# Seven diagonal products in place of a seven-tap sum: the side channels of tiles 0 and 1, and two main taps of tile 1, move from VectorE to TensorE

## The chip, the core and the metric

The kernel is one program on one core of a Trainium2 chip. The metric is the device time of the slowest (here the only) core, in microseconds (us). The kernel before took 2252.99 us (median of 3 runs, 2252.92 to 2253.04). An engine is called by its name or by the short name of the profile: TensorE (PE, its weight loads PEld), VectorE (DVE), ScalarE (ACT), SyncE (SP, which here only issues transfers).

## The reference

`x` is (4, 4096, 192) float32. Layer 0 is a causal convolution with 7 taps, where each of 8 heads (24 channels each) has its own taps; layers 1 and 2 are two token-wise two-matrix networks with 2048 inner features.

```python
w = exp(weight - max(weight)); w = w / (sum(w) + 1e-9)      # (8 heads, 7 taps)
y0[b, s, h, g] = sum_k w[h, k] * x_padded[b, s + k, h, g]    # 6 zeros ahead of each sequence
h1 = y0 @ w_in;   y1 = (h1 * cos(h1)) @ w_out                # 192 -> 2048 -> 192
h2 = relu(y1 @ w2_in); out = (h2 * h2) @ w2_out              # 192 -> 2048 -> 192
```

## The kernel before

The 16384 tokens are 32 tiles of 512. A tile has 192 channels: 128 main channels on 128 partitions, and 64 side channels, whose 512 tokens are folded into two halves of 256 on the upper and the lower 64 partitions. So the convolution's sum of one tile is `conv`, 128 x 768: 512 columns of main channels (`conv_main`) and 256 of side channels (`conv_side`). VectorE makes it in seven instructions (`tap`): a product for tap 0, then six multiply-adds, each of which reads the one before.

TensorE works in float32r. For accuracy each operand is split into a high part and the rest (`x_hi`, `x_lo`, `up_hi`, `up_lo` and so on): ScalarE copies the high part, VectorE subtracts it to get the low part, and products high by high, high by low and low by high are summed. Inner features are taken in eight pairs of 128 per layer. Layer 1 is called "A", layer 2 "B"; a slot is one pair of one layer, and a tile has 16 slots. In a slot TensorE makes `h` (the "up" products) for this pair and adds the pair of four slots before to `y_A` or `y_B` (the "down" products). TensorE uses the upper and the lower 64 rows of its array at once, for different products, the lower ones some steps behind. `h` has two buffers, so the up products of a slot wait until ScalarE has copied `h` of the slot two before (`taken`). The down products of a pair wait for its low part (`lo_made`).

The order on each engine is written by hand, in `turns` and `body`: turn i handles layer 1 of tile i, layer 2 of tile i-1 and the convolution of tile i+1. Turn -1 is the opening: the convolution of tile 0 and the split of layer 1's first weights. Turn 0 has layer 1 alone (slots 3 to 10 hold A 0 to A 7; `FIRST_SLOTS`), with the convolution of tile 1 spread over slots 4 to 10 (`FIRST_TAP_SLOTS`). From turn 1 on both layers run; turns 3 to 30 are a hardware loop.

In an A slot VectorE does, in this order: `low_part` of the slot two before, `times_cosine` of the slot before, the tap of this slot, `fraction` (two instructions) of this slot. ScalarE does `high_part` of the slot two before, the sine (`turned_cosine`) of the slot before, and `read_h` of this slot. In turn 0, slots 11 to 15 hold only the down products of A 4 to A 7.

`on_zeros` are products with a zeroed operand into `y_B`, whose result nobody reads: 42 + 12 in the opening (`WARM_UP`; the 12 wait for the seventh tap of tile 0), and 8 each ahead of the down products of A 5 and A 6 in turn 0 (`FILL`). The sums `y_B` of layer 2 are first used in turn 1.

In the opening ScalarE splits the first part of layer 1's up weights (512 of 2048 columns), then `x` of tile 0 (`split_x1_main`, `split_x1_side`), then the second part (1536 columns). The first up product waits for VectorE's `split_x1` (`x1_made`).

Of the kernel before, what the change touches and what calls it, by code (L numbers as in the profile page):

```python
# [44 lines left out]
FIRST_TAP_SLOTS = (4, 5, 6, 7, 8, 9, 10)  # L45
# [13 lines left out]
WARM_UP, FILL = (42, 12), {5: 8, 6: 8}  # L59
# [58 lines left out]
def tile_program(nc, x, taps_in, w1i, w1o, w2i, w2o, out):  # L118
# [15 lines left out]
    with ExitStack() as ctx:  # L134
# [51 lines left out]

        stage_in_side = sb("stage_in_side", [P, F])
# [9 lines left out]
        taps_loaded = sem("taps_loaded")  # L197
        wi_loaded = (sem("wi_loaded_0"), sem("wi_loaded_1"))
# [6 lines left out]
        taps_exp = sem("taps_exp")  # L205
        wi_hi = sem("wi_hi")
        wi_lo = sem("wi_lo")
        late_hi_made = sem("late_hi_made")
        late_lo = sem("late_lo")
        even_made = sem("even_made")  # L210


# [42 lines left out]
        def _(sp):  # L255
# [33 lines left out]
            sp.wait_ge(tap_done, 2 * K)  # L289
            load_x(2)  # L290
# [19 lines left out]
        def _(pe):  # L310
# [4 lines left out]
            def up_waits(turn, s, kind, p):  # L315
# [140 lines left out]

            def body(turn):
                if turn.first:
                    pe.wait_ge(zeroed, 2)
                    on_zeros(WARM_UP[0])  # L460
                    pe.wait_ge(tap_done, K)
                    on_zeros(WARM_UP[1])
                    return
                for s, (kind, p) in enumerate(turn.slots()):
# [17 lines left out]
        def _(act):  # L482
            act.dma_start(taps[:, :], taps_in).then_inc(taps_loaded, 16)

# [4 lines left out]
            act.activation(unused[:, :], quarter[:, :], ACT.Sin)  # L489

            def layer1_hi_side(part):
                act.wait_ge(wi_loaded[part], 48)
                a, b = (0, FIRST_PART) if part == 0 else (FIRST_PART, F)
                act.activation(up_side["A"][:, a:b], stage_in_side[:, a:b], ACT.Copy).then_inc(wi_hi, 1)
                even = stage_in_side[hi_rows["A"], a:b].rearrange("p (c n m) -> p c n m", n=PAIR, m=P)
                act.activation(up_even[hi_rows["A"], a // (PAIR * P):b // (PAIR * P), :], even[:, :, 0, :], ACT.Copy)
# [80 lines left out]
            def split_x1_side(turn):  # L577

                x_side = xin_side["A"]
                act.activation(x_side[top, halves[0]], conv_side[top, :], ACT.Copy)  # L580
                act.activation(x_side[low, halves[1]], conv_side[low, :], ACT.Copy).then_inc(x1_hi, 1)
                act.activation(x_side[low, halves[0]], conv_side[top, :], ACT.Copy)
                act.activation(x_side[top, halves[1]], conv_side[low, :], ACT.Copy).then_inc(x1_hi, 1)

            def body(turn):
                if turn.first:
                    layer1_hi_side(0)
                    layer1_hi_main(0)
                    split_x1_main(turn)
                    split_x1_side(turn)  # L590
                    layer1_hi_side(1)
                    layer1_hi_main(1)
                    return
# [34 lines left out]
        def _(dve):  # L628
# [72 lines left out]
            def tap(turn, k):  # L701
                done = (turn.i + 1) * K + k
                if k == 0:
# [4 lines left out]
                    dve.tensor_scalar(conv_parts, parts[:, :, 0:HALF_TOK], taps[:, 0:1], None, ALU.mult)\  # L708
# [3 lines left out]
                dve.scalar_tensor_tensor(out=conv_parts, in0=parts[:, :, k:k + HALF_TOK], scalar=taps[:, k:k + 1],  # L712
# [114 lines left out]
```

## Time and profile before

| | |
|---|---|
| median of 3 runs | 2252.99 us |
| the profiled execution | 2253.41 us |
| its span (first to last instruction) | 2251.1 us |
| mean granted TensorE clock | 0.999 |
| TensorE busy | 2239.1 us (99%) |
| VectorE busy | 1774.6 us (79%) |
| ScalarE busy | 1734.8 us (77%) |

Busy time is the share of the span in which an engine had an instruction in work. The chain that ended last is followed back from the last instruction, from each step to what released it: it is 97% TensorE, 2% VectorE, 1% ScalarE. Of VectorE's part nearly all lies in the first 82 us. All starts below are us from the span's start.

### The profile page before, as it was taken

What the parts mean: (1) busy time and instruction counts of PE and PEld (TensorE: products, weight loads), DVE (VectorE), ACT (ScalarE), POOL (GpSimd) and SP (SyncE); (2) the same over time, 40 slices, a digit from 0 to 9 for tenths busy, and PEclk for the clock granted to TensorE, in tenths of its full rate; (3) what the DMA queues carried; (4) which work ended last, traced back from release to release, by engine and by line L of the source; (5) the groups of instructions that cost most, each with busy time, mean ns of one, the idle gap of its engine ahead of it and who ended that gap; (6) DMA issues with size and microseconds to landing.
All of it is one profiled execution on the core that took longest, in us unless ns stands there. A gap on an engine that the chain in (4) does not pass through costs nothing.

```text
span 2251.1 us, 46857 instructions
## 1 busy us (share of the span) xinstructions
PE 2239.1 (99%) x19526; PEld 2213.3 (98%) x19526; DVE 1774.6 (79%) x1813; ACT 1734.8 (77%) x1844; POOL 0.2 (0%) x4
## 2 busy tenths in 40 slices
PE   8999999999999999999999999999999999999999
PEld 7899999999999999999999999999999999999998
DVE  8887788777787777887778877778877788777773
ACT  6677777777877777777778777787777787777876
POOL 0000000000000000000000000000000000000000
PEclk9999999999999999999999999999999999999999
DMA  4000000000000000000000000000000000000000
GB/s 127 27 15 15 9 14 12 10 14 7 14 14 7 14 9 13 14 7 14 14 7 14 14 7 14 7 14 14 7 14 14 7 14 14 7 14 7 7 8 15
DMA packets 13456, 33.26 MB, mean 15 GB/s; under 512 B 1905, under 2 KB 1905, under 8 KB 13169
## 3 DMA queue, kind: packets, MB, share of 16 engines
q1 hardware_dynamic: 13280, 32.81, 4.9%
q8 instruction: 24, 0.39, 0.1%
q14 instruction: 8, 0.06, 0.0%
q10 hardware_dynamic: 144, 0.00, 0.0%
HBM read 20.22 MB, written 12.58 MB: 15 GB/s over the span
## 4 chain that ended last, share of the span: by engine, by line
PE 97%; DVE 2%; ACT 1%; issue 0%; DMA 0%
PE h L346 10%; PE h L350 10%; PE h L348 10%; PE h L352 10%; PE y_A L402 5%; PE y_A L396 5%; PE y_A L400 5%; PE y_A L398 5%; PE y_A L404 5%; PE h L355 5%; PE y_B L400 5%; PE y_B L398 5%; PE y_B L396 5%; PE y_B L404 5%; PE y_B L402 5%; DVE conv L712 0%
## 5 line engine op out<-in xcount | busy, mean ns | idle before, releaser
L698 DVE TENSOR_TENSOR g_lo<-g,g_hi 128x1024 fp32r<-128x1024 f32 x512 | 625.2, 1221 | 272.0 <-ACT g_hi L545 271.1
L545 ACT ACTIVATE g_hi<-g 128x1024 fp32r<-128x1024 f32 x512 | 538.3, 1052 | 44.1 <-DVE g L694 43.4
L537 ACT ACTIVATE w<-w,quarter 128x1024 f32<-128x1024 f32 x256 | 295.5, 1154 | 304.6 <-DVE w L688 304.6
L396 PE MATMUL y_A<-g_hi,dn_lo_A 64*128 64x512 f32 x1024 | 396.9, 388 | 0.1
L402 PE MATMUL y_A<-g_hi,dn_side_A 64*128 64x512 f32 x1024 | 396.3, 387 | 0.0
L398 PE MATMUL y_A<-g_hi,dn_hi_A 64*128 64x512 f32 x1024 | 396.0, 387 | 0.0
L400 PE MATMUL y_A<-g_lo,dn_hi_A 64*128 64x512 f32 x1024 | 395.8, 387 | 0.0
L404 PE MATMUL y_A<-g_lo,dn_side_A 64*128 64x512 f32 x1024 | 395.8, 387 | 0.0
L348 PE MATMUL h<-x_hi_A,up_lo_A 64*128 64x512 f32 x1024 | 394.5, 387 | 0.0
L352 PE MATMUL h<-x_hi_A,up_hi_A 64*128 64x512 f32 x1024 | 394.5, 386 | 0.0
L350 PE MATMUL h<-x_lo_A,up_hi_A 64*128 64x512 f32 x1024 | 394.4, 386 | 0.0
L396 PE MATMUL y_B<-g_hi,dn_lo_B 64*128 64x512 f32 x1000 | 386.6, 387 | 0.0
L398 PE MATMUL y_B<-g_hi,dn_hi_B 64*128 64x512 f32 x1000 | 386.1, 386 | 0.0
L400 PE MATMUL y_B<-g_lo,dn_hi_B 64*128 64x512 f32 x1000 | 386.0, 386 | 0.0
L404 PE MATMUL y_B<-g_lo,dn_side_B 64*128 64x512 f32 x992 | 382.9, 386 | 0.0
L402 PE MATMUL y_B<-g_hi,dn_side_B 64*128 64x512 f32 x992 | 382.9, 386 | 0.0
L352 PE MATMUL h<-x_hi_B,up_hi_B 64*128 64x512 f32 x992 | 382.9, 386 | 0.0
L348 PE MATMUL h<-x_hi_B,up_lo_B 64*128 64x512 f32 x992 | 382.9, 386 | 0.0
L350 PE MATMUL h<-x_lo_B,up_hi_B 64*128 64x512 f32 x992 | 382.9, 386 | 0.0
L694 DVE TENSOR_TENSOR g<-w,g 128x1024 f32<-128x1024 f32 x256 | 313.7, 1225 | 22.7 <-ACT w L537 1.2
L688 DVE SCALAR_TENSOR_TENSOR w<-w,g 128x1024 f32<-128x1024 f32 x256 | 313.7, 1225 | 8.8
L528 ACT ACTIVATE g<-h 128x1024 f32<-128x1024 f32 x256 | 262.2, 1024 | 70.2 <-PE h L352 59.5
(122 smaller groups left out, 6180.0 us busy)
## 6 DMA issues: line engine op xcount, KB each, us to landing
xt<-x SPq DMA_DIRECT2D x32, 393.0 KB, 3.1
out<-late SPq DMA_DIRECT2D x32, 256.0 KB, 2.0
out<-late SPq DMA_DIRECT2D x32, 128.0 KB, 2.3
late<-w_out SPq DMA_DIRECT2D x2, 1536.0 KB, 9.5
stage_in_side<-w_in SPq DMA_DIRECT2D x2, 512.0 KB, 4.2
stage_in_side<-w_in SPq DMA_DIRECT2D x4, 256.0 KB, 5.3
w<-w_in SPq DMA_DIRECT2D x1, 768.0 KB, 7.1
stage_in_side<-w_in SPq DMA_DIRECT2D x2, 384.0 KB, 9.1
```

The source lines that it names most:

```text
L348: mm = pe.matmul(dst, up_lo[kind][rows, f], x_hi[rows, :], start=False, stop=z)
L350: mm = pe.matmul(dst, up_hi[kind][rows, f], x_lo[rows, :], start=False, stop=z)
L352: mm = pe.matmul(dst, up_hi[kind][rows, f], x_hi[rows, :], start=False, stop=z)
L396: mm = pe.matmul(sums[:, 0, :], dn_lo[kind][rows, c, :], hi, start=a, stop=False)
L398: mm = pe.matmul(sums[:, 0, :], dn_hi[kind][rows, c, :], hi, start=False, stop=False)
L400: mm = pe.matmul(sums[:, 0, :], dn_hi[kind][rows, c, :], lo, start=False, stop=z)
L402: mm = pe.matmul(sums[:, 1, :], dn_side[kind][rows, c, :], hi, start=a, stop=False)
L404: mm = pe.matmul(sums[:, 1, :], dn_side[kind][rows, c, :], lo, start=False, stop=z)
L545: act.activation(g_hi[:, s % RING, :, :], g[:, s % RING, :, :], ACT.Copy).then_inc(hi_made[kind], 1)
L688: dve.scalar_tensor_tensor(out=v, in0=v, scalar=ROUND, in1=u, op0=ALU.subtract, op1=ALU.subtract).then_inc(frac, 1)
L694: dve.tensor_tensor(u, v, u, ALU.mult).then_inc(g_made, 1)
L698: dve.tensor_tensor(g_lo[:, r, :, :], g[:, r, :, :], g_hi[:, r, :, :].bitcast(F32), ALU.subtract).then_inc(lo_made[kind], 1)
```

## The change

TensorE makes part of the convolution with diagonal matrices. ScalarE, after an identity matrix has been loaded (one more transfer, 128 x 128 float32, issued by ScalarE into `y_side`), writes seven scaled copies `diag[:, k, :]`, each with tap k of every channel on its diagonal. A product of `diag[:, k, :]` with the shifted columns of `x` is tap k. These operands are plain float32, not float32r.

- Tile 0: the 256 side columns are seven such products, in TensorE's opening (`side_taps(0)`), into bank 1 of `y_B`; VectorE's seven taps cover 512 columns.
- Tile 1: the 256 side columns are seven products after the up products of slot 5 (`side_taps(1)`); taps 0 and 1 of the 512 main columns are two products after slot 6 (`main_taps`), into bank 0 of `y_B`. VectorE's taps 0 and 1 (slots 4 and 5) go; its tap 2 (slot 6, `tap_on_sums`) reads the sum in PSUM and writes `conv`; all five that are left cover 512 columns.
- Zero products in the opening: 14, then the seven side products, then 6, then (after the seventh tap) 12. `FILL` stays at 8 and 8.
- ScalarE's opening order: seven diagonal copies, then the high parts of the first weights with `up_even` last, then the side split (it waits for `conv_made`), then the main split, then the second part of the weights, again with `up_even` last. A semaphore `wi_even` covers `up_even`.

```diff
-FIRST_TAP_SLOTS = (4, 5, 6, 7, 8, 9, 10)
+PE_TAPS = 2
+FIRST_TAP_SLOTS = (None, None, 6, 7, 8, 9, 10)
-WARM_UP, FILL = (42, 12), {5: 8, 6: 8}
+WARM_UP, FILL = (14, 6, 12), {5: 8, 6: 8}
+        conv_pe, conv_pe_side = y["B"][:, 0, :], y["B"][:, 1, 0:HALF_TOK]
+        ident, diag = y_side[:, 0:P], sb("diag", [P, K, P])
             sp.wait_ge(tap_done, K)
+            sp.wait_ge(conv_made, 1)
             load_x(1)
             sp.wait_ge(wi_lo, 4)
+            sp.wait_ge(wi_even, 2)
             load_layer2_up(0)
...
+            def side_taps(t):
+                pe.wait_ge(x_loaded, (t + 1) * 16)
+                for k in range(K):
+                    if t == 0:
+                        pe.wait_ge(diag_made, k + 1)
+                    mm = pe.matmul(conv_pe_side, diag[:, k, :], parts[:, 2, k:k + HALF_TOK],
+                                   start=k == 0, stop=k == K - 1)
+                mm.then_inc(conv_made, 1)
+            def main_taps():
+                for k in range(PE_TAPS):
+                    mm = pe.matmul(conv_pe.rearrange("p (s n) -> p s n", s=2), diag[:, k, :],
+                                   parts[:, 0:2, k:k + HALF_TOK], start=k == 0, stop=k == PE_TAPS - 1)
+                mm.then_inc(conv_made, 1)
...
+                        if turn.peeled and turn.i == 0 and p == 2:
+                            side_taps(1)
+                        if turn.peeled and turn.i == 0 and p == 3:
+                            main_taps()
...
             act.dma_start(taps[:, :], taps_in).then_inc(taps_loaded, 16)
+            act.dma_start(ident, identity).then_inc(ident_loaded, 16)
...
+            act.wait_ge(ident_loaded, 16)
+            act.wait_ge(taps_step, 6)
+            for k in range(K):
+                act.activation(diag[:, k, :], ident, ACT.Copy, scale=taps[:, k:k + 1]).then_inc(diag_made, 1)
...
                 if turn.first:
                     layer1_hi_side(0)
                     layer1_hi_main(0)
+                    layer1_hi_even(0)
+                    split_x1_side(turn)
                     split_x1_main(turn)
-                    split_x1_side(turn)
...
+            def tap_on_sums():
+                k = PE_TAPS
+                dve.wait_ge(conv_made, 3)
+                dve.wait_ge(x1_hi, 3)
+                dve.wait_ge(x1_made, 1)
+                dve.scalar_tensor_tensor(out=conv_parts[:, 0:2, :], in0=parts[:, 0:2, k:k + HALF_TOK],
+                                         scalar=taps[:, k:k + 1],
+                                         in1=conv_pe.rearrange("p (s n) -> p s n", s=2),
+                                         op0=ALU.mult, op1=ALU.add).then_inc(tap_done, k + 1)
```

ScalarE, from the load of the taps to the second part of the weights. Before:

```order
L489 ACTIVATE unused<-quarter 128x1 [waits zeroed]
L494 ACTIVATE up_side_A<-stage_in_side 128x512 [waits wi_loaded_0]
L496 ACTIVATE up_even<-stage_in_side 64x256
L500 ACTIVATE up_hi_A<-w 128x512
L575 ACTIVATE x_hi_A<-conv 128x512 [waits tap_done]
L580 ACTIVATE x_side_A<-conv 64x256
L581 ACTIVATE x_side_A<-conv 64x256
L582 ACTIVATE x_side_A<-conv 64x256
L583 ACTIVATE x_side_A<-conv 64x256
L494 ACTIVATE up_side_A<-stage_in_side 128x1536 [waits wi_loaded_1]
```

The same stretch of ScalarE now (`y_side` holds the identity):

```order
L533 ACTIVATE diag<-y_side,taps 128x128 [waits taps_step,ident_loaded]
L533 ACTIVATE diag<-y_side,taps 128x128 x6
L538 ACTIVATE up_side_A<-stage_in_side 128x512 [waits wi_loaded_0]
L548 ACTIVATE up_hi_A<-w 128x512
L543 ACTIVATE up_even<-stage_in_side 64x256
L630 ACTIVATE x_side_A<-y_B 64x256 [waits conv_made]
L631 ACTIVATE x_side_A<-y_B 64x256
L632 ACTIVATE x_side_A<-y_B 64x256
L633 ACTIVATE x_side_A<-y_B 64x256
L623 ACTIVATE x_hi_A<-conv 128x512 [waits tap_done]
L538 ACTIVATE up_side_A<-stage_in_side 128x1536 [waits wi_loaded_1]
```

Seven copies stand ahead of the weights, and the side split stands ahead of the main one, behind a wait for TensorE.

TensorE in turn 0, from the last up products of slot 5 (A 2) to the first of slot 6 (A 3), before:

```order
L350 MATMUL h<-x_lo_A,up_hi_A 128x512
L352 MATMUL h<-x_hi_A,up_hi_A 128x512
L346 MATMUL h<-x_side_lo,up_side_A 128x512 [waits taken_A]
L348 MATMUL h<-x_hi_A,up_lo_A 128x512
L350 MATMUL h<-x_lo_A,up_hi_A 128x512
```

The same place of TensorE now (`diag` and `xt` are the float32 operands), and behind it the place between slot 6 and the first products of slot 7 (A 4):

```order
L367 MATMUL h<-x_lo_A,up_hi_A 128x512
L369 MATMUL h<-x_hi_A,up_hi_A 128x512
L479 MATMUL y_B<-xt,diag 128x256 [waits x_loaded]
L479 MATMUL y_B<-xt,diag 128x256 x6
L363 MATMUL h<-x_side_lo,up_side_A 128x512 [waits taken_A]
L365 MATMUL h<-x_hi_A,up_lo_A 128x512
```

```order
L369 MATMUL h<-x_hi_A,up_hi_A 128x512
L485 MATMUL y_B<-xt,diag 128x512 x2
L363 MATMUL h<-x_side_lo,up_side_A 128x512 [waits lo_made_A,late_lo,taken_A]
L413 MATMUL y_A<-g_hi,dn_lo_A 128x512
L365 MATMUL h<-x_hi_A,up_lo_A 128x512
```

Nine float32 products came in; nothing of TensorE's other work changed places.

VectorE in turn 0 at slots 4 to 6, before and now (`conv<-xt,taps` is tap 0, L712 and L767 are later taps; the instruction ahead of a tap is `times_cosine`, the one behind it starts `fraction`):

```order
L694 TENSOR_TENSOR g<-w,g 128x1024 [waits cosine]
L708 TENSOR_SCALAR conv<-xt,taps 128x768 [waits x1_made,x1_hi,x_loaded]
L686 TENSOR_SCALAR w<-g 128x1024 [waits taken_A]
L688 SCALAR_TENSOR_TENSOR w<-w,g 128x1024 [waits whole]
L663 SCALAR_TENSOR_TENSOR dn_side_A<-late,dn_side_A 128x16x64 [waits late_hi_made]
L698 TENSOR_TENSOR g_lo<-g,g_hi 128x1024 [waits hi_made_A]
L694 TENSOR_TENSOR g<-w,g 128x1024 [waits cosine]
L712 SCALAR_TENSOR_TENSOR conv<-xt,taps,conv 128x768 [waits tap_done]
L686 TENSOR_SCALAR w<-g 128x1024 [waits taken_A]
```

```order
L747 TENSOR_TENSOR g<-w,g 128x1024 [waits cosine]
L739 TENSOR_SCALAR w<-g 128x1024 [waits taken_A]
L741 SCALAR_TENSOR_TENSOR w<-w,g 128x1024 [waits whole]
L751 TENSOR_TENSOR g_lo<-g,g_hi 128x1024 [waits hi_made_A]
L747 TENSOR_TENSOR g<-w,g 128x1024 [waits cosine]
L781 SCALAR_TENSOR_TENSOR conv<-xt,taps,y_B 128x512 [waits x1_hi,x1_made,conv_made]
L739 TENSOR_SCALAR w<-g 128x1024 [waits taken_A]
L741 SCALAR_TENSOR_TENSOR w<-w,g 128x1024 [waits whole]
L751 TENSOR_TENSOR g_lo<-g,g_hi 128x1024 [waits hi_made_A]
```

The taps of slots 4 and 5 are gone, and the tap of slot 6 reads `y_B` and has 512 columns.

## Rows read from the trace of the kernel before

**Rows 1.** The page: busy time, share and count of each engine.

```profile
PE 2239.1 (99%) x19526; PEld 2213.3 (98%) x19526; DVE 1774.6 (79%) x1813; ACT 1734.8 (77%) x1844; POOL 0.2 (0%) x4
```

**Rows 2.** Windows: stretch, length, busy (count) by engine, clock, DMA share, GB/s.

```profile
0.00:5.00 5.00, 3.52 (x8) 2.81 (x9) 1.03 (x5) 1.69 (x3) 0.20 (x4) 1.00 0.55 167
...
30.00:35.00 5.00, 3.59 (x20) 3.50 (x22) 4.96 (x6) 2.15 (x3) 0.00 (x0) 0.74 0.79 285
...
100.00:110.00 10.00, 10.00 (x92) 8.27 (x90) 8.58 (x10) 8.72 (x11) 0.00 (x0) 1.00 0.00 0
```

**Rows 3.** Timeline of the opening, VectorE and ScalarE: start, duration, what [idle before <-releaser].

```profile
5.61 1.02 DVE L708 TENSOR_SCALAR conv<-xt,taps 128x768 f32<-128x768 f32 x1
6.10 0.20 ACT L489 ACTIVATE unused<-quarter 128x1 f32<-128x1 f32 x1
6.66 6.29 DVE L712 SCALAR_TENSOR_TENSOR conv<-xt,taps,conv 128x768 f32<-128x768 f32 x6
7.34 0.63 ACT L494 ACTIVATE up_side_A<-stage_in_side 128x512 fp32r<-128x512 f32 x1 [1.04 <-DMA stage_in_side<-w_in]
...
12.98 0.63 ACT L575 ACTIVATE x_hi_A<-conv 128x512 fp32r<-128x512 f32 x1 [3.92 <-DVE conv L712]
...
14.80 0.42 ACT L583 ACTIVATE x_side_A<-conv 64x256 fp32r<-64x256 f32 x1
...
15.24 1.49 ACT L494 ACTIVATE up_side_A<-stage_in_side 128x1536 fp32r<-128x1536 f32 x1
15.33 0.42 DVE L722 TENSOR_TENSOR x_side_lo<-conv,x_side_A 64x256 fp32r<-64x256 f32 x1
...
19.13 1.76 DVE L654 TENSOR_TENSOR up_lo_A<-w,up_hi_A 128x1536 fp32r<-128x1536 f32 x1 [0.61 <-ACT up_hi_A L500]
...
20.92 0.69 DVE L686 TENSOR_SCALAR w<-g 128x1024 f32<-128x1024 f32 x1
```

**Rows 4.** Tile stage_in_side: its transfers' issue times, and us to landing.

```profile
L262 SPq DMA_DIRECT2D stage_in_side<-w_in x4: 466/584/685, 1.6 to 4.0; - x4
...
DMA to landing us min/median/max: 3.8/5.2/10.0
```

**Rows 5.** Timeline of TensorE, from the last zero products to slot 7.

```profile
13.00 2.60 PEld L455 LDWEIGHTS y_B<-x_side_last 128*128 128x128 f32 x12 [0.47 <-DVE conv L712]
...
15.95 0.49 PE L346 MATMUL h<-x_side_lo,up_side_A 64*128 64x512 f32 x1
...
18.48 0.50 PE L346 MATMUL h<-x_side_lo,up_side_A 64*128 64x512 f32 x1
...
24.20 0.39 PE L352 MATMUL h<-x_hi_A,up_hi_A 64*128 64x512 f32 x1
...
31.41 0.46 PE L346 MATMUL h<-x_side_lo,up_side_A 64*128 64x512 f32 x1 [2.79 <-DVE g_lo L698]
```

**Rows 6.** Timeline of turn 0, VectorE and ScalarE, slots 7 and 8.

```profile
40.69 1.23 DVE L698 TENSOR_TENSOR g_lo<-g,g_hi 128x1024 fp32r<-128x1024 f32 x1 [0.26 <-ACT g_hi L545]
...
46.94 1.01 ACT L528 ACTIVATE g<-h 128x1024 f32<-128x1024 f32 x1
...
48.21 1.01 DVE L712 SCALAR_TENSOR_TENSOR conv<-xt,taps,conv 128x768 f32<-128x768 f32 x1
49.14 0.69 DVE L686 TENSOR_SCALAR w<-g 128x1024 f32<-128x1024 f32 x1
```

**Rows 7.** Timeline of TensorE, slot 10 to the end of turn 0's down products.

```profile
48.00 0.50 PE L346 MATMUL h<-x_side_lo,up_side_A 64*128 64x512 f32 x1 [0.74 <-ACT g L528]
...
52.66 0.49 PE L402 MATMUL y_A<-g_hi,dn_side_A 64*128 64x512 f32 x1
...
66.09 0.39 PE L400 MATMUL y_A<-g_lo,dn_hi_A 64*128 64x512 f32 x1
66.64 0.47 PE L396 MATMUL y_A<-g_hi,dn_lo_A 64*128 64x512 f32 x1
...
69.58 0.39 PE L400 MATMUL y_A<-g_lo,dn_hi_A 64*128 64x512 f32 x1
```

More of the change, by code:

```diff
@@ L115, in before, with tile_program @@
                 return None
-def tile_program(nc, x, taps_in, w1i, w1o, w2i, w2o, out):
+def tile_program(nc, x, taps_in, identity, w1i, w1o, w2i, w2o, out):
     TILES, _, WIDTH = x.shape
@@ L210, in tile_program @@
         even_made = sem("even_made")
+        conv_made = sem("conv_made")
         filled = {k: sem(f"filled_{k}") for k in "AB"}
@@ L289, in _ @@
             sp.wait_ge(tap_done, 2 * K)
+            sp.wait_ge(conv_made, 3)
             load_x(2)
@@ L577, in split_x1_side @@
             def split_x1_side(turn):
[L579 to L583, printed above, removed]
+                x_side, sums = xin_side["A"], side_sums(turn)
+                if turn.peeled and turn.i <= 0:
+                    act.wait_ge(conv_made, turn.i + 2)
+                act.activation(x_side[top, halves[0]], sums[top, :], ACT.Copy)
+                act.activation(x_side[low, halves[1]], sums[low, :], ACT.Copy).then_inc(x1_hi, 1)
+                act.activation(x_side[low, halves[0]], sums[top, :], ACT.Copy)
+                act.activation(x_side[top, halves[1]], sums[low, :], ACT.Copy).then_inc(x1_hi, 1)
             def body(turn):
@@ L707, in tap @@
                         dve.wait_ge(x1_made, turn.i + 1)
-                    dve.tensor_scalar(conv_parts, parts[:, :, 0:HALF_TOK], taps[:, 0:1], None, ALU.mult)\
+                    sums, held = conv_of(turn)
+                    dve.tensor_scalar(sums, held[:, :, 0:HALF_TOK], taps[:, 0:1], None, ALU.mult)\
                        .then_inc(tap_done, 1)
@@ L711, in tap @@
                 dve.wait_ge(tap_done, done)
[L712 to L723 removed]
+                sums, held = conv_of(turn)
@@ new lines, in tap, with conv_of @@
+                dve.scalar_tensor_tensor(out=sums, in0=held[:, :, k:k + HALF_TOK], scalar=taps[:, k:k + 1],
+                                         in1=sums, op0=ALU.mult, op1=ALU.add).then_inc(tap_done, 1)
+            def conv_of(turn):
+                n = 2 if turn.peeled and turn.i <= 0 else 3
+                return conv_parts[:, 0:n, :], parts[:, 0:n, :]
+            def tap_on_sums():
[7 more added lines that the diff above has]
+                                         op0=ALU.mult, op1=ALU.add).then_inc(tap_done, k + 1)
@@ new lines, in split_x1 @@
+            def split_x1(turn):
+                x_side, sums, to = xin_side["A"], side_sums(turn), lo_rows["A"]
+                if not turn.first:
+                    dve.wait_ge(x1_hi, turn.i * 3 + 4)
+                    dve.tensor_tensor(xin_lo["A"][:, :], conv_main, xin_hi["A"][:, :].bitcast(F32), ALU.subtract)
+                dve.wait_ge(x1_hi, turn.i * 3 + (6 if turn.peeled and turn.i == 0 else 5))
+                dve.tensor_tensor(xin_side_lo[to, halves[0]], sums[top, :],
+                                  x_side[top, halves[0]].bitcast(F32), ALU.subtract)
+                done = dve.tensor_tensor(xin_side_lo[to, halves[1]], sums[low, :],
+                                         x_side[low, halves[1]].bitcast(F32), ALU.subtract)
+                if turn.first:
+                    dve.wait_ge(x1_hi, 3)
+                    done = dve.tensor_tensor(xin_lo["A"][:, :], conv_main, xin_hi["A"][:, :].bitcast(F32),
+                                             ALU.subtract)
+                done.then_inc(x1_made, 1)
@@ L775, in body @@
                         if turn.runs("C") and s == taps_at[k]:
-                            tap(turn, k)
+                            if turn.peeled and turn.i == 0 and k == PE_TAPS:
+                                tap_on_sums()
+                            else:
+                                tap(turn, k)
                     if kind == "A" and turn.runs("A"):
@@ L817 @@
     arrays = {
-        "x": x_tiles, "tap_rows": tap_rows, "w1_in": moe_w_in[channels], "w1_out": down(moe_w_out),
+        "x": x_tiles, "tap_rows": tap_rows, "identity": np.eye(P, dtype=np.float32), "w1_in": moe_w_in[channels], "w1_out": down(moe_w_out),
         "w2_in": moe2_w_in, "w2_out": down(moe2_w_out),
```

25 lines of the change are left out of this document (15 added, 10 removed).

## The prediction, made before the changed kernel had run

> **What bounds the kernel now.** I read the page first, then windows over the first 200 us, then the timelines of the opening and of turn 0. TensorE is busy for 99% of the span [rows 1], and from about 91 us on it has no gap: in 100 to 110 it is busy for 10.00 of 10.00 us at the full clock [rows 2]. Nothing in the change touches the turns behind that, so the change can only move the time at which TensorE becomes full, and what it moves there goes into the total one for one. Ahead of it there are two runners. VectorE makes tile 0's seven taps from 5.61 to 12.98, and ScalarE, VectorE and TensorE follow in a row until TensorE starts its first up product at 15.95 [rows 3, 5]. Then a loop of VectorE and ScalarE sets the pace of turn 0: in slots 7 and 10 TensorE waits for them, 2.79 and 0.74 us [rows 5, 7]. The last down products of turn 0 end at 69.58 + 0.39 = 69.97 [rows 7]; turn 1 starts from there. I follow the changed kernel to that point.
>
> **The opening.** VectorE: six taps of 768 columns take 6.29 us, with the small gap to the next instruction 1.053 each, the first 1.05 [rows 3]. A multiply-add of 1024 columns does not stand in the rows, but a subtraction of 1024 takes 1.23 [rows 6] and a tap of 768 takes 1.01 to 1.02, so a column costs some 1.0 ns; 256 fewer take away 0.27, leaving 0.77 to 0.79. I take 0.77: seven are 5.4, and the taps end at 11.0 instead of 12.98.
>
> ScalarE: free at 6.30 [rows 3]. A copy costs (1.49 - 0.63)/1024 = 0.84 ns per column [rows 3], so one of 128 columns 0.63 - 384 x 0.84 ns = 0.31. The scale is read from a tile, and a 256-column copy takes 0.42; bounds are 0.31 and 0.42 per diagonal, I take 0.38. The last diagonal is there at 9.0. High parts of the first weights: 0.63 + 0.63 + 0.42 and gaps, to 10.75. Then the side split, 4 x 0.42, to 12.45, if TensorE's sums are there; then the main split 0.63 (the taps are done since 11.0), to 13.08. VectorE ends its side subtractions at 13.3 and the main one (0.69) at 14.05. Before, the last subtraction ended at 15.75 and the first product started 0.2 later, so it now starts at 14.25.
>
> TensorE: what one float32 product costs stands in no row. In float32r 512 columns take 2.60/12 = 0.217 alone [rows 5], and 0.2275 in the stream of pairs for upper and lower rows (10 us hold 92 products, edges counted, so some 44 pairs) [rows 2]. Lower bound: one pass, 256 columns = 0.11 us. Upper bound: four passes, each with its weight load of 0.18 to 0.22 laid open, 4 x (0.114 + 0.18) = 1.18. The kernel itself needs high and low parts of both operands for a float32 result; all four part-products of 256 columns are 4 x 0.114 = 0.455, with weight loads hidden as in the zero products, where a 0.217 load lies beside each 0.217 product [rows 5]. I take x = 0.455 per 256 columns, 2x per 512. The Trainium skill, "FP8 and Floating Point Precision", TensorE Precision Notes, says that true FP32 takes 4 passes through the array; by it the sum is the one below. The page "TensorE: Matmul & The Clock Gate", Part 3, The mechanism, says that weight loads overlap running matmuls only where the row group differs; our zero products use all rows and overlap with their loads all the same, so the trace speaks against it, and by it x would be at the upper bound.
>
> 14 zero products from 1.49: eight in the first 5 us at half the later rate [rows 2], six more to 6.3. Side products from 6.75 (first diagonal) to 6.75 + 7x = 9.95, ahead of ScalarE's 10.75, so nothing waits. Six zeros, to 11.25, twelve more, to 13.9: before 14.25, with 0.35 to spare. That cover is gone when x > 0.51; from there TensorE starts 7(x - 0.51) later.
>
> **Layer 1's second weights and turn 0's loop.** ScalarE's second part may start at 13.08 instead of 15.24, but the last of its loads is issued at 4.0 and the longest landing is 10.0 [rows 4]: 14.0. Then 1.49 + 1.49 us of copies, VectorE's two subtractions of 1.76 behind them, end 19.2, not 20.89. The `h` of A 0 is full at 14.25 + 3.6 = 17.85, read by 19.0. VectorE's first `fraction` starts at 19.2 instead of 20.92: gain 1.7. Bounds: 2.0 if only the products count, 0 if the load came just before 15.24.
>
> In the loop a tap stands between `times_cosine` and `fraction`, 48.21 to 49.14: 0.93 [rows 6]. The sine of the next slot waits for `fraction`, so a tap is in the period in full. Two taps go: 1.86. Five get 0.27 shorter, but in slot 6 the loop runs through ScalarE, which makes the high part of layer 2's up weights and already holds VectorE for 0.26 [rows 6]: four count, 1.08. Together with the opening VectorE's loop is earlier by 1.7 + 1.86 + 1.08 = 4.65 at its end.
>
> **TensorE in turn 0.** Slots 3, 4, 5 start 2.53 apart [rows 5]. The last product of slot 5 leaves the rows free 3.42 after the slot's start (24.20 + 0.23 against 21.01). Then 7x, slot 6 with 3.42 again, two products 4x, and 0.1 for the switch. Slot 7 starts at
>
> 14.25 + 5.06 + 3.42 + 0.1 + 3.42 + 11x = 26.25 + 11x = 31.25,
>
> against 31.41 before: TensorE fills its wait of 2.79 [rows 5] and the clock need not fall, which was 0.74 in 30 to 35 [rows 2]. Its inputs are there: it waits for the low part of A 0, ready just before 31.41, now 1.7 + 0.93 earlier, 28.7. Nobody waits for it: ScalarE reads `h` of A 5 from 46.94 [rows 6], now from 43.1, that of A 4 one slot of 5.2 sooner, about 38. The sum of the main taps is there at 31.2; the tap of slot 6 stands two slots ahead of that of slot 8 (48.21 [rows 6]), so at 37.6 before and 34.0 now.
>
> From slot 7 TensorE goes on without a wait: three slots of 4.43, 4.33 and 4.33 (19 steps of 0.2275, the first a little longer), to slot 10 at 44.3. That slot also waits for `h` of A 5, read by 47.95 before [rows 6], now by 47.95 - 1.7 - 1.86 - 0.27 = 44.1. From slot 10 to the end of turn 0's down products it was 21.97, with 0.3 of wait at 66.3 (66.09 + 0.23 to 66.64, [rows 7]); the two times eight zeros are in it. So it is 21.67, and the end is at 44.3 + 21.67 = 66.0 against 69.97: gain 4.0. The down products of A 7 started at 66.64 behind VectorE; by VectorE alone they would be 4.65 earlier, with an end at 65.3. So TensorE, with its zeros, sets the end now, by 0.7 us. Turn 1 follows as before: the split of its x hangs on VectorE's loop, which is earlier still.
>
> **Small edits.** The identity is 64 KB; at 167 to 285 GB/s [rows 2] that is 0.2 to 0.4 us for whoever queues behind it, inside my margin for the 14.0. It must land by 6.3, 5 us after issue. SP's new waits (`conv_made`, `wi_even`) end before the ones beside them. The wait ahead of `FILL` is over by then. Queued behind ScalarE's wait for `conv_made` are the main split and the second weights; that is the price of a large x.
>
> Profiled: 2253.41 - 4.0 = 2249.4. That execution lies 0.42 above the median of 2252.99, so I predict 2249.0.
>
> **The rivals.**
> 1. *More than that.* ScalarE's diagonals at 0.31 and weights that land by 13.1: first product at 13.75, slot 7 at 30.7, A 5 read by 43.4; end 65.2 and gain 4.8: 2248.2. For it: the median landing is 5.2, not 10. Against it: both must hold.
> 2. *The second weights bind.* They land at 15.2: `fraction` keeps its 20.92, A 5 is read by 45.8, end 67.5, gain 2.5: 2250.5. An identity that lands late, or a clock that falls once in the opening for some 3 us, gives about the same. For it: ScalarE never waited for this load before, so nothing but its landing time [rows 4] says when it came. Against: by that time it came at 14.0 at the latest.
> 3. *Two weight loads laid open in a product*, x = 0.455 + 2 x 0.184 = 0.82: first product at 16.4, slot 7 at 37.4. The end is where it was for a slot 7 at 69.97 - 21.67 - 13.1 = 35.2, so it is 2.2 later: 2255.2.
> 4. *All four laid open*, x = 1.18: first product 18.95, slot 7 at 43.9, 8.7 later: 2261.7. It is one mechanism, the price of a float32 product, and it decides from x = 0.70: 14.25 + 7(x - 0.51) + 12.0 + 11x = 35.2. For 3 and 4: this kernel has no float32 product, and its half-row loads of 0.184 are longer than a 256-column pass of 0.114, so they cannot hide behind one pass each. Against: a load hides if two passes share it.
> If a product took one pass (0.11), the gain would be no more than 4.2, since A 5 and the zeros then set the end.
>
> **How the numbers follow.** Forecast (2248.6 to 2249.6) 0.50; rival 1 0.17; rival 2 0.15; rival 3 0.11; rival 4 0.07. A measurement of this kernel tells some 0.2% from no change, 4.5 us: faster means under 2248.5, slower over 2257.5. Faster has rival 1 and an edge of the forecast, 0.20; slower has rival 4, 0.07; within, the rest, 0.73. The range runs from 2247.9, below rival 1, to 2252.5, above rival 2, and leaves out rivals 3 and 4, 0.18.
>
> **What would show it.** Right: taps of 0.77, first up product at 14.2, `fraction` of A 0 at 19.2, slot 7 near 31.3 without a wait, clock 1.00 in 30 to 35, no wait ahead of the down products of A 7, their end near 66.0, and the same distance from there to the last instruction. Wrong: the float32 products' pitch away from 0.455, ScalarE idle behind its first `up_even`, a wait of ScalarE for the second weights beyond 14.0, or zeros that end after `x` is split. If the end of turn 0 is 4 us earlier and the total is not, the cause lies in turn 1.

## The result, and the profile after

The changed kernel takes 2249.41 us (median of 22 runs, 2249.13 to 2250.03), the kernel before 2253.31 us (22 runs, 2252.92 to 2254.43). The ratio is 0.9983, 95% interval 0.9976 to 0.9989: 3.9 us faster, within 0.2%. The forecast was 2249.0, with a range of 2247.9 to 2252.5.

The page of the changed kernel, its line of busy times (before: [rows 1]):

```profile
PE 2240.2 (100%) x19536; PEld 2212.7 (98%) x19536; DVE 1769.9 (79%) x1811; ACT 1736.4 (77%) x1851; POOL 0.2 (0%) x4
```

TensorE has 10 products more: 22 zero products less (42 to 14 + 6 in the opening), and 32 records for the 16 float32 products, two each. The span went from 2251.1 to 2247.6.

Windows of the changed kernel, columns as in [rows 2]:

```profile
0.00:5.00 5.00, 3.52 (x8) 2.82 (x9) 0.87 (x4) 1.49 (x2) 0.20 (x4) 1.00 0.61 186
...
30.00:35.00 5.00, 5.00 (x34) 3.28 (x34) 4.85 (x6) 4.19 (x5) 0.00 (x0) 1.00 0.53 221
...
100.00:110.00 10.00, 10.00 (x92) 8.29 (x90) 8.88 (x9) 7.53 (x8) 0.00 (x0) 1.00 0.01 2
```

In 30 to 35 TensorE is busy for 5.00 us, not 3.59, and its granted clock is 1.00, not 0.74. In 100 to 110 it is as busy as before, 10.00 us at 1.00.

The opening of the changed kernel, timelines of VectorE and ScalarE (start, duration, what, idle before; answers to [rows 3]):

```profile
5.79 0.49 DVE L762 TENSOR_SCALAR conv<-xt,taps 128x512 f32<-128x512 f32 x1
6.32 4.69 DVE L767 SCALAR_TENSOR_TENSOR conv<-xt,taps,conv 128x512 f32<-128x512 f32 x6
11.04 0.69 DVE L704 TENSOR_TENSOR up_side_A<-stage_in_side,up_side_A 64x512 fp32r<-64x512 f32 x1
11.76 0.69 DVE L707 TENSOR_TENSOR up_lo_A<-w,up_hi_A 128x512 fp32r<-128x512 f32 x1
12.37 0.41 DVE L794 TENSOR_TENSOR x_side_lo<-y_B,x_side_A 64x256 fp32r<-64x256 f32 x1
12.79 0.43 DVE L796 TENSOR_TENSOR x_side_lo<-y_B,x_side_A 64x256 fp32r<-64x256 f32 x1
13.23 0.69 DVE L800 TENSOR_TENSOR x_lo_A<-conv,x_hi_A 128x512 fp32r<-128x512 f32 x1
...
19.02 0.69 DVE L739 TENSOR_SCALAR w<-g 128x1024 f32<-128x1024 f32 x1 [0.89 <-ACT g L576]
```

```profile
6.40 2.14 ACT L533 ACTIVATE diag<-y_side,taps 128x128 f32<-128x128 f32 x7
...
10.23 0.38 ACT L630 ACTIVATE x_side_A<-y_B 64x256 fp32r<-64x256 f32 x1 [0.21 <-PE y_B L479]
...
11.82 0.63 ACT L623 ACTIVATE x_hi_A<-conv 128x512 fp32r<-128x512 f32 x1
13.07 1.49 ACT L538 ACTIVATE up_side_A<-stage_in_side 128x1536 fp32r<-128x1536 f32 x1 [0.62 <-DMA stage_in_side<-w_in]
```

The taps end at 11.0; the side split waits 0.21 for TensorE; `x` is split at 13.23 + 0.69 = 13.92, with VectorE at work without a wait from the taps to there; the second weights land at 13.0, and ScalarE waits 0.62 for them. VectorE's loop starts at 19.02 (before 20.92).

TensorE in the changed kernel, from the opening to the end of turn 0's down products (answers to [rows 5, 7]; L479 are the side products, L485 the main taps, L472 the zeros):

```profile
6.93 3.26 PE L479 MATMUL y_B<-xt,diag 128*128 128x256 f32 x14
9.84 4.48 PE L472 MATMUL y_B<-x_side_last 128*128 128x512 f32 x18
14.25 0.49 PE L363 MATMUL h<-x_side_lo,up_side_A 64*128 64x512 f32 x1
...
22.84 2.43 PE L479 MATMUL y_B<-xt,diag 128*128 128x256 f32 x10
...
26.06 0.50 PE L363 MATMUL h<-x_side_lo,up_side_A 64*128 64x512 f32 x1
...
29.59 1.99 PE L485 MATMUL y_B<-xt,diag 128*128 128x512 f32 x4
31.51 0.49 PE L363 MATMUL h<-x_side_lo,up_side_A 64*128 64x512 f32 x1
...
44.58 0.39 PE L363 MATMUL h<-x_side_lo,up_side_A 64*128 64x512 f32 x1
...
62.53 0.39 PE L417 MATMUL y_A<-g_lo,dn_hi_A 64*128 64x512 f32 x1
63.08 0.47 PE L413 MATMUL y_A<-g_hi,dn_lo_A 64*128 64x512 f32 x1
...
66.01 0.39 PE L417 MATMUL y_A<-g_lo,dn_hi_A 64*128 64x512 f32 x1
```

There is no bracket with a releaser any more: TensorE waits for nobody from 14.25 to the end of turn 0. The end is 66.01 + 0.39 = 66.40 against 69.97, 3.57 earlier. From there on nothing moved: the last product of the kernel starts 2176.1 us after turn 0's last down product in one trace (69.58 to 2245.70) and 2176.2 in the other (66.01 to 2242.19).

Whether TensorE still waits for VectorE ahead of the last down products, those of A 7, is seen from VectorE's low part of A 7, before and now:

```profile
65.22 1.23 DVE L698 TENSOR_TENSOR g_lo<-g,g_hi 128x1024 fp32r<-128x1024 f32 x1 [1.21 <-ACT g_hi L545]
```

```profile
60.40 1.23 DVE L751 TENSOR_TENSOR g_lo<-g,g_hi 128x1024 fp32r<-128x1024 f32 x1 [1.21 <-ACT g_hi L593]
```

Before, it was made at 66.45, and the products started at 66.64 [rows 7]. Now it is made at 61.63 and they start at 63.08, 1.45 later: VectorE is ahead.

### The profile page after: what moved, and what is told of

It is laid out like the page before. It is cut to its first block, busy times and chain, and to the rows that moved or that the text cites. A ratio compares the mean times of both kernels' runs of the same rounds, so it can differ in the third digit from the quotient of the medians.

```text
span 2247.6 us, 46890 instructions
## 1 busy us (share of the span) xinstructions
PE 2240.2 (100%) x19536; PEld 2212.7 (98%) x19536; DVE 1769.9 (79%) x1811; ACT 1736.4 (77%) x1851; POOL 0.2 (0%) x4
## 4 chain that ended last, share of the span: by engine, by line
PE 99%; DVE 0%; ACT 0%; issue 0%; ACTq 0%
PE h L363 10%; PE h L367 10%; PE h L369 10%; PE h L365 10%; PE y_A L419 5%; PE y_A L413 5%; PE y_A L417 5%; PE y_A L415 5%; PE y_A L421 5%; PE h L372 5%; PE y_B L417 5%; PE y_B L415 5%; PE y_B L413 5%; PE y_B L421 5%; PE y_B L419 5%; PE y_B L472 1%
## 5 line engine op out<-in xcount | busy, mean ns | idle before, releaser
L593 ACT ACTIVATE g_hi<-g 128x1024 fp32r<-128x1024 f32 x512 | 538.9, 1053 | 44.3 <-DVE g L747 43.5
```

The costliest lines, as they stand in the source:

```text
L593: act.activation(g_hi[:, s % RING, :, :], g[:, s % RING, :, :], ACT.Copy).then_inc(hi_made[kind], 1)
```

## The experiments

Each kernel was timed beside the kernel before, whose medians there were 2253.26 (both parts alone, both kernels without zeros), 2253.16 (4 and 7 zeros, the doubled set, three taps with all zeros, four taps) and 2253.30 (the last three). The second group ran on another chip than the other two. So a difference between two of these kernels carries an uncertainty of some 0.15 us from that alone. All ratios are to the kernel before. Theory T: in the changed kernel TensorE's own chain, from its first up product through turn 0, sets the end of turn 0, and VectorE's loop is 1.2 to 1.7 us ahead. Theory V: VectorE's loop still sets it.

**The opening's part alone.** Tile 1 is convolved as before; what reads or waits for its sums follows.

```diff
-FIRST_TAP_SLOTS = (None, None, 6, 7, 8, 9, 10)
+FIRST_TAP_SLOTS = (4, 5, 6, 7, 8, 9, 10)
...
-                            side_taps(1)
...
-                            main_taps()
...
```

> Only the opening's part of the change: tile 0's side channels are made by TensorE, tile 1 keeps its seven 768-column taps on VectorE. My theory (in the changed kernel TensorE's own work, from its first up product at 14.25 to the last down product of turn 0 at 66.4, sets the end; here VectorE's loop sets it again): the loop starts 1.9 us earlier (19.0 instead of 20.9) and carries that through, so turn 0's down products end near 68.1 and the total is 2253.3 - 1.9 = 2251.4. Rival (the two parts add up fully, with the opening worth the 2.0 us that the taps get shorter): the same 2251.3 here, so this run alone does not tell; it does together with the run of the other half. Rival (the opening is hidden, because the second weights' transfer starts the loop): 2253.

Measured: 2251.14, ratio 0.9990 (0.9981 to 0.9999), gain 2.1. VectorE's loop starts at 18.89. TensorE waits again ahead of slot 7, as before the change; its timeline:

```profile
29.39 0.76 PE L362 MATMUL h<-x_side_lo,up_side_A 64*128 64x512 f32 x1 [2.78 <-DVE g_lo L746]
...
45.97 0.50 PE L362 MATMUL h<-x_side_lo,up_side_A 64*128 64x512 f32 x1 [0.73 <-ACT g L571]
```

They are 2.02 and 2.03 earlier than in [rows 5, 7]: here VectorE's loop sets the pace, and the 2.03 that it starts earlier arrives whole. The rival in which the second weights hide the opening is out.

**Turn 0's part alone.** Tile 0 is convolved as before, with 42 + 12 zeros; the diagonals stand behind the first weights, the main split ahead of the side split again (the cut shows the opening alone).

```diff
-WARM_UP, FILL = (14, 6, 12), {5: 8, 6: 8}
+WARM_UP, FILL = (42, 0, 12), {5: 8, 6: 8}
...
-                    side_taps(0)
...
```

> Only turn 0's part: tile 0 stays on VectorE with 42 + 12 zero products, the diagonals are made by ScalarE behind the first weights, where it idled; tile 1 is as in the changed kernel. My theory (TensorE sets the end): first up product at 15.95, slot 7 17.3 later at 33.2, end of turn 0's down products 34.9 after that at 68.1, total 2253.3 - 1.9 = 2251.4, though VectorE's loop is 2.9 earlier. Rival (VectorE's loop sets the end in this part, as it did before): gain 2.9, 2250.4.

Measured: 2251.22, ratio 0.9992 (0.9983 to 1.0001), gain 2.0. The interval just reaches 1, but the slowest run (2251.80) lies below the fastest of the kernel before beside it (2252.95). V asked for a gain of 2.9. Its last down product of turn 0 in the timeline of TensorE:

```profile
67.71 0.38 PE L416 MATMUL y_A<-g_lo,dn_hi_A 64*128 64x512 f32 x1
```

The end is 68.09, where T put it (68.1). The parts are 2.1 and 2.0, together 4.1 against 3.9 for the whole. That they nearly add up is no sign that each does one thing: the first is worth 2.0 to VectorE's loop or 1.7 to TensorE, the second 2.9 to VectorE's loop or 1.9 to TensorE.

**The changed kernel without zeros in turn 0**, and **the kernel before without them**, each with this edit:

```diff
-{5: 8, 6: 8}
+{}
```

> The changed kernel without the sixteen zero products in turn 0. My theory: TensorE's own work incl. these 16 (4.1 us) sets the end, 1.2 to 1.6 us behind what VectorE's low parts would allow: with the clock at full speed the end of turn 0's down products goes from 66.4 to about 64.9 and the total to 2247.9. Rival (the end hangs on VectorE's loop): no change, 2249.4. Rival (the zeros hold the clock): with gaps of 1.0 and 1.6 us ahead of the down products of A 5 and A 6 the granted clock falls in 55 to 65 and the total is 2250 to 2252.

> The kernel before without the sixteen zero products of turn 0. If they were hidden behind VectorE's loop there, as I hold, they are worth no more than 0.3 us: 2253.0. If they also set the end before: 1.5 us or more, 2251.8. If they hold the clock: slower, 2254 to 2256.

Measured, changed kernel without zeros: median 2250.51, and eleven times in three groups, 2247.66 to 2247.76 (three), 2249.86 to 2250.68 (four), 2252.08 to 2252.26 (four). So both the first theory and the clock rival came in, in different runs of one kernel. The mean granted clock goes with the groups: 1.0 in the first, 0.998 to 0.999 in the second, 0.997 to 0.998 in the third. Lowest against lowest (2249.13) the first group is 1.5 under the changed kernel: what the zeros cost it. The profiled run (2250.68) is of the middle group. Its timeline of TensorE and its windows:

```profile
52.86 0.49 PE L413 MATMUL y_A<-g_hi,dn_lo_A 64*128 64x512 f32 x1 [0.75 <-DVE g_lo L751]
57.83 0.49 PE L413 MATMUL y_A<-g_hi,dn_lo_A 64*128 64x512 f32 x1 [1.61 <-DVE g_lo L751]
```

```profile
50.00:55.00 5.00, 4.25 (x28) 3.11 (x27) 4.88 (x6) 3.52 (x4) 0.00 (x0) 1.00 0.00 0
55.00:60.00 5.00, 3.39 (x22) 2.53 (x21) 3.97 (x4) 2.24 (x3) 0.00 (x0) 0.97 0.24 82
60.00:65.00 5.00, 4.85 (x19) 3.46 (x16) 4.52 (x6) 2.18 (x6) 0.00 (x0) 0.50 0.01 3
```

TensorE waits 0.75 and 1.61 us for low parts; then the granted clock is 0.50 (1.2 GHz) in 60 to 65.

The kernel before without zeros: median 2254.06, 2252.75 to 2257.09. Its lowest is 0.2 under the lowest of before (2252.95 beside it), where T had 0.3. That alone is weak, since its clock is lower than that of the kernel before in most of its runs (0.996 to 0.998 against 0.998 to 0.999), the fastest included. Its trace says the same more directly. The down products of A 6 start, with the zeros and without them:

```profile
63.11 0.50 PE L396 MATMUL y_A<-g_hi,dn_lo_A 64*128 64x512 f32 x1
```

```profile
62.75 0.79 PE L396 MATMUL y_A<-g_hi,dn_lo_A 64*128 64x512 f32 x1 [0.59 <-DVE g_lo L698]
```

That is 0.36, and the rest of the zeros' time is a wait for VectorE. So before the change the zeros lay beside a wait and cost 0.2 to 0.4; in the changed kernel they cost 1.5, because most of that wait is gone.

**Fewer zeros, so that they end when the low parts come.**

```diff
-{5: 8, 6: 8}
+{5: 4, 6: 7}
```

> The changed kernel with 4 and 7 zero products instead of 8 and 8, so that they end where VectorE's low parts of A 5 and A 6 arrive (52.9 and 57.9). My theory: turn 0's down products end 1.1 to 1.4 us earlier and, as no gap is left, the clock stays full in every run: 2248.1, with a narrow spread. Rival (it is the number of zeros, not the gap, that holds the clock): spread as in the run without zeros, up to 2252. Rival (the zeros cost nothing): 2249.4.

Measured: 2248.53 (2247.99 to 2248.83), ratio 0.9979 (0.9970 to 0.9988), 0.9 under the changed kernel, and all its runs are faster than all of the changed kernel's. The profiled span is 2246.4, 1.2 shorter, as T has it; the median is 0.4 above T's 2248.1. Timeline of TensorE, then its window:

```profile
52.12 1.19 PE L472 MATMUL y_B<-x_side_last 128*128 128x512 f32 x4
...
56.55 1.89 PE L472 MATMUL y_B<-x_side_last 128*128 128x512 f32 x7
58.36 0.49 PE L413 MATMUL y_A<-g_hi,dn_lo_A 64*128 64x512 f32 x1
```

```profile
60.00:65.00 5.00, 4.85 (x35) 3.97 (x34) 4.45 (x6) 2.25 (x6) 0.00 (x0) 1.00 0.00 0
```

No wait, clock 1.00, no time above 2249. So it is the gap that matters, not the number of zeros. Which of the two gaps brings the clock down, or whether it takes both, was not tried.

**The price of a float32 product**: tile 1's side products made twice.

```diff
                             side_taps(1)
+                            side_taps(1)
...
```

What waits for the sums counts one more signal.

> The changed kernel with tile 1's seven side products made twice (the second set overwrites the first with the same values): the price of a float32 product by itself. My theory: a product of 256 columns costs 0.42, seven cost 2.9, all of it on the chain, since TensorE sets the end: 2252.3. Rival (hidden, as TensorE used to wait 2.8 us ahead of slot 7): 2249.4. Rival (h of A 4 comes late too and adds to it): up to 2253.3.

Measured: 2252.23 (2252.06 to 2253.04), 2.8 over the changed kernel by the medians, 3.0 when each is taken against the kernel before beside it; T had 2.9. Timeline of TensorE:

```profile
22.56 6.31 PE L479 MATMUL y_B<-xt,diag 128*128 128x256 f32 x28
28.80 0.49 PE L363 MATMUL h<-x_side_lo,up_side_A 64*128 64x512 f32 x1
```

From 22.56 to 28.80 are 6.24 us for fourteen products, 3.22 for seven in the changed kernel (22.84 to 26.06): (6.24 - 3.22)/7 = 0.43 each. The room that TensorE had ahead of slot 7 was used up by the first set; the second set is on the chain one for one.

**Three main taps on TensorE, zeros kept.**

```diff
-PE_TAPS = 2
-FIRST_TAP_SLOTS = (None, None, 6, 7, 8, 9, 10)
+PE_TAPS = 3
+FIRST_TAP_SLOTS = (None, None, None, 6, 7, 8, 9)
```

> The changed kernel with three main taps of tile 1 on TensorE instead of two (VectorE's four left stand in slots 6 to 9), with both times eight zero products kept. My theory (TensorE's chain sets the end, VectorE's loop is 1.2 to 1.7 us ahead): one more 512-column float32 product costs 0.85 to 0.95 and VectorE's 0.66 less is worth nothing: 2250.3. Rival (VectorE's loop still sets the end): 2248.8.

Measured: 2250.34 (2249.95 to 2250.84), 0.9 slower than the changed kernel (1.1 against the kernel before beside each), as T has it; V is out by 1.5 us. VectorE's tap less is worth nothing here.

**Three main taps and 0 and 4 zeros**, and **four main taps and no zeros**:

```diff
-PE_TAPS = 2
-FIRST_TAP_SLOTS = (None, None, 6, 7, 8, 9, 10)
-{5: 8, 6: 8}
+PE_TAPS = 3
+FIRST_TAP_SLOTS = (None, None, None, 6, 7, 8, 9)
+{6: 4}
```

```diff
-PE_TAPS = 2
-FIRST_TAP_SLOTS = (None, None, 6, 7, 8, 9, 10)
-{5: 8, 6: 8}
+PE_TAPS = 4
+FIRST_TAP_SLOTS = (None, None, None, None, 6, 7, 8)
+{}
```

> Three main taps of tile 1 on TensorE, and 0 and 4 zero products in turn 0 instead of 8 and 8. My theory (max of two chains): slot 7 at 32.4, TensorE's chain without the zeros' surplus, VectorE's low parts of A 6 at 57.3 and A 7 at 61.0, end of turn 0's down products at 64.2 instead of 66.4: 2247.2, to 2247.6 as with four taps, and a narrow spread since no gap is over 0.3 us. Rival (only the kernel with no wait at all holds its clock): spread to 2250.

> Four main taps of tile 1 on TensorE (two more float32 products of 0.96 with 1.9 us together), VectorE's three left in slots 6 to 8, and no zero products in turn 0: work takes the place of the zeros. My theory: slot 7 starts at 33.4, the down products of A 5 at 54.0 (low part at 52.3, no wait), those of A 6 and A 7 follow without a gap, the end is 63.9 instead of 66.4, the clock stays full: 2246.9, with a narrow spread. Rival (slot 7 at 33.4 fills h of A 4 at 37.8, when ScalarE reads it at 37.86, so the loop slips): 2247.5 to 2248. Rival (float32 products do not hold the clock as the zeros do): spread up to 2250 and more.

Measured: 2247.98 (2247.22 to 2248.69) and 2247.46 (2247.20 to 2247.75), ratios 0.9976 (0.9967 to 0.9985) and 0.9975 (0.9965 to 0.9984). With four taps I had 2246.9 and missed by 0.6. Slot 7 came at 33.32 as expected (33.4), but each stretch of down products behind it takes 3.45, not 3.2; TensorE's timeline has their starts (A 5, A 6, A 7), VectorE's the low part of A 7:

```profile
54.18 0.49 PE L419 MATMUL y_A<-g_hi,dn_side_A 64*128 64x512 f32 x1
...
57.63 0.49 PE L419 MATMUL y_A<-g_hi,dn_side_A 64*128 64x512 f32 x1
...
61.09 0.49 PE L419 MATMUL y_A<-g_hi,dn_side_A 64*128 64x512 f32 x1
```

```profile
59.18 1.23 DVE L751 TENSOR_TENSOR g_lo<-g,g_hi 128x1024 fp32r<-128x1024 f32 x1 [1.21 <-ACT g_hi L593]
```

The time is that of the rival with a slipping loop (2247.5 to 2248), but its mechanism did not come in: the low part of A 7 is there at 60.41, 0.68 before the products that need it, and TensorE waits for none.

The profiled spans of the two kernels are the same, 2245.6, and the medians of all their spans are 2245.7 and 2245.55; so most of the 0.5 between them lies outside the span. With three taps I had 2247.2 to 2247.6 and a narrow spread, and missed both: the median is 2247.98, the times differ by up to 1.5 us. In the spans they differ by 0.9 only (2245.4 to 2246.3), as in the changed kernel (2247.3 to 2248.2); the rest is time outside the span, 1.8 to 2.9 us. Their mean granted clock is 0.999 or 1.0 in all eleven runs, so the rival that has it fall is out. The windows of the kernel with four taps where the kernel without zeros had fallen:

```profile
55.00:60.00 5.00, 4.85 (x33) 3.92 (x30) 3.71 (x4) 3.05 (x5) 0.00 (x0) 1.00 0.01 3
60.00:65.00 5.00, 4.85 (x35) 4.00 (x34) 4.21 (x6) 1.66 (x4) 0.00 (x0) 1.00 0.00 0
```

Useful float32 products ahead of slot 7 take the place of the zeros behind it: nothing is left to wait for, and the clock stays.

**Two zeros less in the opening**, alone, and with four taps and no zeros in turn 0:

```diff
-WARM_UP, FILL = (14, 6, 12), {5: 8, 6: 8}
+WARM_UP, FILL = (14, 6, 10), {5: 8, 6: 8}
```

(With four taps the last set is `{}`, and `PE_TAPS` and `FIRST_TAP_SLOTS` are those of four taps.)

> The changed kernel with 10 instead of 12 zero products behind VectorE's seventh tap. In every trace so far the first up product starts 0.35 after the weight load of the last zero product has ended (before: 15.60 to 15.95; changed: 13.90 to 14.25), and 0.2 to 0.6 after x is split. My theory: these zeros, not the split of x, set the first up product; two less start it 0.1 to 0.4 earlier, and as TensorE's chain sets the end the total gains the same: 2249.2 (2249.0 to 2249.3). Rival (the split of x sets it): 2249.4. Rival (the clock falls in the gap): later by 1 us or more in some runs.

> Four main taps on TensorE, no zero products in turn 0, and 10 instead of 12 zeros in the opening. My theory: the gains of both add up, since TensorE's chain has no wait from its first up product on: 2247.46 minus 0.2 to 0.4, so 2247.2. Rival (with four taps something else sets the end, ScalarE reading h of A 4): 2247.5.

Measured: 2249.22 (2249.02 to 2249.50) and 2247.08 (2246.93 to 2247.47). The steps of 0.2 and 0.4 (0.5 when each of the two kernels with four taps is taken against the kernel before beside it) lie in the expected direction and size, but the single runs of the first overlap with those of the changed kernel, so it alone shows little. Nor does its trace: the first up product starts at 14.11, and in the kernels with twelve zeros at 13.97 to 14.84 (see the opening, below). Weight loads of TensorE around the first up product, changed kernel, then the one with four taps and ten zeros:

```profile
11.89 2.01 PEld L472 LDWEIGHTS y_B<-x_side_last 128*128 128x128 f32 x9
14.25 0.18 PEld L363 LDWEIGHTS h<-x_side_lo,up_side_A 64*128 64x128 f32 x1 [0.35 <-issue]
```

```profile
12.00 1.32 PEld L472 LDWEIGHTS y_B<-x_side_last 128*128 128x128 f32 x6
13.89 0.18 PEld L363 LDWEIGHTS h<-x_side_lo,up_side_A 64*128 64x128 f32 x1 [0.58 <-issue]
```

In the first, the up product follows the zeros' last weight load by 0.35. In the second `x` is split at 13.82 and that load has been over since 13.32: the split sets it. The last kernel is the fastest of all, 2247.08 against 2253.30, ratio 0.9973 (0.9962 to 0.9983), and 2.3 under the changed kernel.

## Why the prediction was right, and where its sum was off

*The opening.* First up product 14.25 forecast, 14.25 measured: that exact hit is luck. The terms cancel, and one of them varies from one execution to the next. The taps ended at 11.0 as forecast, starting 0.18 later, with 0.79 per multiply-add instead of 0.77 and 0.53 for the first instead of 0.77. (The weights of the taps landed 0.19 later. The identity's transfer behind theirs does not explain it: with the same two transfers the taps started at 5.46 to 5.70 in the other kernels, at 5.61 before.) ScalarE's diagonals came every 0.29, not 0.38, so ScalarE was through with the first weights at 10.02, not 10.75, and then waited 0.21 for TensorE's side sums. `x` was split at 13.92, not 14.05, and by another chain than mine: VectorE makes five subtractions back to back behind its last tap, from 11.04 to 13.92. "The zeros end with 0.35 to spare" was wrong: their weight loads end at 13.90, and the first up product follows 0.35 later, at 14.25. That 0.35 stands in the trace of before, too (15.60 to 15.95), where I had read the start as 0.2 behind the split of `x`, and in every profiled kernel with twelve zeros there. So the zeros set the start, and the threshold of x = 0.51 for a dearer product had been reached already.

So from its first zero product at 1.49 on, TensorE's opening is one chain, and its length is not fixed. The first 14 zero products took 5.11 to 6.30 us in the eight profiled kernels with this opening and twelve zeros at its end (5.54 in the changed kernel), and the first up product started at 13.97 to 14.84; the shortest goes with the earliest and the longest with the latest. Before the change the zeros waited 0.47 us for the seventh tap [rows 5], which hid such differences.

Both conditions of rival 1 came in, diagonals below 0.31 and weights that landed by 13.1, but not its first product at 13.75, since neither sets the start. Three of my signs of a wrong forecast came in as well: products at 0.43 and not 0.455, ScalarE idle behind its first `up_even` (0.21), and zeros that end after `x` is split (9.84 + 4.48 = 14.32 against 13.92). By the numbers above, none of the three moved the end by more than 0.3 us.

*The price of a float32 product.* I took 0.455 per 256 columns; it is 0.43 (the doubled set), and 0.86 per 512: four main taps last 3.63 (29.69 to 33.32), three 2.78. Each product stands in the trace as two weight loads and two products, 14 for seven; each of the two takes 0.215, the time of two passes of 256 columns. The Trainium skill, "FP8 and Floating Point Precision", TensorE Precision Notes, has four passes for true FP32; the trace agrees, since four passes of 256 columns are 4 x 0.1085 = 0.43 by the rate of the zeros (0.217 per 512). The Trainium skill's page "TensorE: Matmul & The Clock Gate", Part 3, The mechanism, says in one place that weight loads overlap running products only where the row group differs, and just above it names a background weight buffer as a second case. The trace contradicts the first: the loads of 0.19 use all rows and are hidden. Rivals 3 and 4 rested on loads laid open: both are refuted.

*The loop.* `fraction` of A 0 at 19.2 forecast, 19.02 measured, set by `h` (0.89 of wait for ScalarE) and not by the weights, which landed at 13.0, not 14.0: rival 2 is out. A tap in the loop takes 0.67 to the next instruction (54.14 to 54.81), 0.66 forecast. By the low part of A 7 (66.45 before, 61.63 now) VectorE's loop is 4.82 earlier at its end, 4.65 forecast.

*Turn 0.* Slot 7 at 31.25 forecast, 31.51 measured. I had counted 0.1 for the switches between half-row and whole-row products; there are four in turn 0, 0.09 into and 0.20 out of each of its two groups of float32 products, together 0.6. The cheaper products give back 0.27 (4.74 for 5.01). Slot 10 at 44.3 forecast, 44.58 measured. The end at 66.0 forecast, 66.40 measured: besides the 0.28 that slot 10 is late, I had taken 0.3 off for a wait at 66.3 that was none, and 0.15 of the two came back, nearly all of it before the first zeros, as slot 10 no longer starts behind a wait. In the changed kernel the low part of A 7 is made at 60.40 + 1.23 = 61.63, and the same gap stands there, 62.53 + 0.23 to 63.08. A gap of 0.30 to 0.32 stands ahead of A 7's down products in the kernels with 4 and 7 zeros and with four taps as well; it goes with the start of a stretch of down products, and what makes it was not tried. So the gain up to this point is 3.6, not 4.0.

*The time.* The gain is 3.9 by the medians, 4.0 forecast. The profiled pair (2253.41 and 2249.42) differs by 4.0, but only 3.5 of it lies in the span; 0.5 lies outside, 2.3 us before (2253.41 - 2251.1) and 1.8 after. The spans of all timed runs say 3.75: median 2251.3 for 89 runs of the kernel before beside the experiments, 2247.55 for 22 of the changed kernel, so the profiled execution of before (2251.1) was one with a short span. The forecast of 2249.0 is 0.4 low, of which 0.3 has nothing to do with the change: I had carried the 0.42 between the profiled execution and the median of three runs as a constant, and the median of 22 runs is 0.3 higher than that of the three. The other 0.1 is the gain.

*That TensorE now sets the end* is the step on which the small gain rests, and it is shown from four sides: the parts alone, the third tap, the doubled set and the zeros. Only the margin was mis-sized: I gave 0.7 us, the runs without zeros show 1.5, and the low part of A 7 lies 1.45 ahead of its products. Of the difference, 0.4 is TensorE's own lateness, 0.2 lies between the low part of A 7 before (66.45) and the start that I had read as VectorE's (66.64), and 0.2 is the loop.

## What to carry to other kernels

When an engine gets work into a wait, the wait was also what hid everything else that it did there: zeros that had cost 0.2 to 0.4 us cost 1.5 afterwards, so re-measure the fillers with the change. Write both chains to the same end and take the later, for each part; two parts that add up may do so by different chains. And look twice at an idle time without a named releaser: twice here (0.35 ahead of the first up product, 0.3 ahead of A 7) it stayed when nobody was waited for any more. And when the last wait of a chain is gone, what varied ahead of it from run to run, here the first zero products, reaches everything behind it.

## What the runs showed of the hardware that I had not expected

- The clock fell after waits of 0.75 and 1.61 us with 3.4 us of products between them, and it did so in some runs and not in others of one kernel: mean granted clocks from 1.0 down to 0.997 and times from 2247.66 to 2252.26, where kernels without such gaps spread by 0.5 to 1.5.
- A multiply by a per-partition tap took 0.49 us for 128x512 and 1.02 for 128x768 ([rows 3]), while the multiply-adds went from 1.02 to 0.75. Why the first is so much cheaper was not tried.
- Seven copies of 128 columns took 0.386 each but started every 0.29; ScalarE's reads of 256 columns took 0.38 from PSUM and 0.40 to 0.42 from SBUF.
- The time outside the span is 1.7 to 2.0 us in most runs, but not in all: in 20 of the 89 runs of the kernel before it is above 2.0, up to 3.07, in the 22 of the changed kernel 1.74 to 1.92. With gains of a few us in 2250, this is as large as some of the steps compared here, so the spans should be compared beside the times.
- The first zero products run at half the later pace (eight in 3.52 us, 0.44 each, against 0.217), with the window's clock at 1.00 [rows 2]. The clock column does not show this slow start.
